# Ahead of the first MLP: the turns, the reciprocals and the value products one slot sooner, into the accumulators' banks

## What is computed

```python
scores = scale * np.matmul(q, k.transpose(0, 1, 3, 2))
kth = np.partition(scores, -top_k, axis=-1)[..., -top_k:-top_k + 1]   # top_k = 32
scores = np.where(scores >= kth, scores, -1000000000.0)
scores = scores - np.max(scores, axis=-1, keepdims=True)
attn = np.exp(scores)
attn = attn / (np.sum(attn, axis=-1, keepdims=True) + 1e-09)
x = np.matmul(attn, v)                                  # -> (2304, 512)
x = (sigmoid(x @ w_gate) * (x @ w_val)) @ w_out         # 512 -> 1536 -> 512
out = relu(x @ w_in) ** 2 @ w2_out                      # 512 -> 2048 -> 512
```

## Time and profile before

| | |
|---|---|
| median of 3 runs | 1231.99 us (1231.97 to 1233.85) |
| profiled execution | 1234.21 us, its span 1232.4 us |
| PE, busy in the span | 1164.7 us, 95% |
| DVE, busy in the span | 848.1 us, 69% |
| ACT, busy in the span | 740.2 us, 60% |
| POOL, busy in the span | 627.4 us, 51% |

### The profile page before, as it was taken

The page is one execution under the profiler, slowest core; times in us unless marked ns, Lnnn a source line. Parts: engine busy times, 40 slices in busy tenths (PEclk is TensorE's granted clock), DMA queues, the critical chain, the costliest instruction groups (busy, mean ns, idle before and its releaser), DMA issues.

```text
span 1232.4 us, 21820 instructions
## 1 busy us (share of the span) xinstructions
PE 1164.7 (95%) x7520; PEld 988.5 (80%) x7520; DVE 848.1 (69%) x1756; ACT 740.2 (60%) x1758; POOL 627.4 (51%) x539
## 2 busy tenths in 40 slices
PE   3459998999999999999999999999999999999999
PEld 1347887889988988888888777777777888888999
DVE  7988997978779967878997677788854544610121
ACT  5877777876778766656775665577554443621231
POOL 4865667766667745445663454356533342530220
PEclk9769999999999999999999999999999999999999
DMA  9874767677666685565556555545555455556997
GB/s 333 317 281 142 253 208 247 220 258 263 212 231 225 231 293 197 166 193 192 167 197 208 209 171 180 184 155 189 171 176 189 166 181 181 178 180 229 364 362 266
DMA packets 89245, 270.13 MB, mean 219 GB/s; under 512 B 9904, under 2 KB 15024, under 8 KB 89136
## 3 DMA queue, kind: packets, MB, share of 16 engines
q1 hardware_dynamic: 89136, 268.74, 63.8%
HBM read 228.33 MB, written 40.37 MB: 218 GB/s over the span
## 4 chain that ended last, share of the span: by engine, by line
PE 80%; ACT 8%; POOL 6%; DVE 3%; issue 2%; DMA 1%; SPq 0%; ACTq 0%; DVEq 0%; POOLq 0%
PE ps L553 21%; PE ps L555 20%; PE ps L554 20%; PE ps L494 7%; PE ps L458 5%; PE ps L474 5%; POOL below L784 3%; PE ps L539 3%; ACT scores L585 2%; DVE work L721 2%; DVE top L719 1%; ACT probs L604 1%; POOL stage L779 1%; ACT below L590 1%; ACT below L597 1%
## 5 line engine op out<-in xcount | busy, mean ns | idle before, releaser
L784 POOL TENSOR_TENSOR below<-scores,below 128x576 f32<-128x576 f32 x144 | 205.4, 1426 | 294.7 <-ACT below L597 291.6
L719 DVE MAX8 top<-work 128x8 f32<-128x576 f32 x432 | 313.0, 752 | 5.0
L553 PE MATMUL ps<-xy_hi,ring 128*128 128x512 f32 (+3 forms) x800 | 291.1, 364 | 0.0
L555 PE MATMUL ps<-xy_hi,ring 128*128 128x512 f32 (+3 forms) x800 | 282.8, 354 | 0.0
L554 PE MATMUL ps<-xy_lo,ring 128*128 128x512 f32 (+3 forms) x800 | 282.5, 353 | 0.0
L721 DVE MATCH_REPLACE8 work<-top,work 128x576 f32<-128x576 f32 x288 | 213.8, 743 | 0.0
L553 PE MATMUL ps<-g_hi,ring 128*128 128x512 f32 (+3 forms) x560 | 203.0, 362 | 0.0
L555 PE MATMUL ps<-g_hi,ring 128*128 128x512 f32 (+3 forms) x560 | 197.8, 353 | 0.0
L554 PE MATMUL ps<-g_lo,ring 128*128 128x512 f32 (+3 forms) x560 | 197.6, 353 | 0.0
L553 PEld LDWEIGHTS ps<-xy_hi,ring 128*128 128x128 f32 x800 | 150.8, 189 | 24.2 <-issue 9.4
L555 PEld LDWEIGHTS ps<-xy_hi,ring 128*128 128x128 f32 x800 | 150.8, 189 | 15.9
(11 more groups left out here) (58 smaller groups left out, 1734.5 us busy)
## 6 DMA issues: line engine op xcount, KB each, us to landing
ring<-w_split SPq DMA_DIRECT2D x318, 512.0 KB, 3.7
wring<-w_in SPq DMA_DIRECT2D x113, 256.0 KB, 4.0
w_split<-stage SPq DMA_DIRECT2D x46, 512.0 KB, 4.3
w_split<-ring SPq DMA_DIRECT2D x22, 512.0 KB, 2.9
vt<-v_in SPq DMA_DIRECT2D x16, 480.0 KB, 5.5
heads_in<-qk_in SPq DMA_DIRECT2D x16, 336.0 KB, 4.4
vt<-v_in SPq DMA_DIRECT2D x16, 320.0 KB, 3.9
heads_in<-qk_in SPq DMA_DIRECT2D x16, 240.0 KB, 4.0
```

Source lines behind the costliest of these rows:

```text
L553: nc.tensor.matmul(dst, w_hi, hi[:, k, 0:WIDTH[c]], start=first, stop=False)
L555: mm = nc.tensor.matmul(dst, w_lo, hi[:, k, 0:WIDTH[c]], start=False, stop=final)
L719: nc.vector.max(out=best, in_=sc if step == 0 else wk).then_inc(sel_step[t % 2], 1)
L784: nc.gpsimd.tensor_tensor(out=below[:, t % 2, :], in0=scores[:, t % PLACES, :], in1=below[:, t % 2, :], op=ALU.subtract).then_inc(mask_don ...
```

## The change

For tiles and units of chunk 0 only, the reciprocal and the normalising move from slot t+3 to t+2, the turn from END+3 to END+2, and the value product from END+4 to END+3. Their turned blocks go into banks 5, 6 and 7, which no MLP uses yet, so these turns no longer wait for copied scores or for the copied product of the unit before, and second-head scores no longer wait for them; the wait for the product moves to `times_v`. `MLP_AT` of chunk 0 becomes slot 15, while that of chunk 1 stays 41: 136 halves are spread over 26 slots where they were over 25.

Within a slot: in the prelude ScalarE now writes sign and enlarged sign ahead of the copy of scores, takes the exponential ahead of `copy_pt` (in slot 14 behind it), and the weight splits follow; 23 splits are spread over slots 0 to 13, one or two in each, and GpSimd does its part a slot later, between mask and normalise. VectorE's reciprocal stands behind the third pair of selection steps in the prelude, and from slot 15 on behind the second pair, where it stood behind the first. Later units keep their slots. The chunks are described by pieces of a batch; they hold the same tokens as before, but the outputs of chunks 3 and 4 are stored by two DMAs for each block of 128 features (8 DMAs more).

```diff
+PIECES = (((0, 0, 3),), ((0, 3, 6),), ((1, 0, 7),), ((1, 7, 2), (2, 0, 6)), ((2, 6, 3), (3, 0, 5)), ((3, 5, 4),))
...
-MASK, NORM, TURN, PROD = 2, 3, 3, 4
-MLP_AT = [CHUNK_END[c] + (5 if c < NW else 6) for c in range(NC)]
+MASK = 2
+MLP_AT = [CHUNK_END[c] + (4 if c == 0 else 6) for c in range(NC)]
+NORM_AT, TURN_AT, PROD_AT = {}, {}, {}
+for _t in range(NT):
+    _late = UNITS[TILES[_t][0]][0] > 0
+    NORM_AT[_t + 2 + _late] = _t
+    if _t in UNIT_AT:
+        TURN_AT[_t + 2 + _late] = PROD_AT[_t + 3 + _late] = UNIT_AT[_t]
...
-    SPLIT_AT.setdefault(min(2, MLP_AT[0] - (NPRE + 1) // 2) + _k // 2, []).append(_k)
+    SPLIT_AT.setdefault(_k * (MLP_AT[0] - 1) // NPRE, []).append(_k)
...
+        def turned(u, k, n):
+            bank = (5 if early(u) else 2) + k // 4
+            return ps[:, bank, P * (k % 4):P * (k % 4 + n)]
...
             def turn(u):
                 pe.wait_ge(norm_done, END[u] + 1)
                 wait(pe, pt_copied, u)
-                wait(pe, s_copied, max([t + 1 for t in range(NT) if TILES[t][1] == 1
-                                        and FIRST_OF[TILES[t][0]] - SCORE <= END[u] + TURN], default=0))
-                wait(pe, x_done, u)
+                if not early(u):
+                    wait(pe, s_copied, max([t + 1 for t in range(NT) if TILES[t][1] == 1
+                                            and FIRST_OF[TILES[t][0]] - SCORE <= TURN_SLOT[u]], default=0))
+                    wait(pe, x_done, u)
...
             def times_v(u):
                 pe.wait_ge(pt_copied, u + 1)
+                if early(u):
+                    wait(pe, x_done, u)
...
+            for s in range(min(SCORE_AT) + 1, MLP_AT[0]):
+                if 0 <= s - MASK:
+                    find_below(s - MASK)
+                    enlarge(s - MASK)
                 if s - 1 in SCORE_AT:
                     for t in tiles_of(SCORE_AT[s - 1]):
                         copy_scores(t)
+                if s in PROD_AT and s == MLP_AT[0] - 1:
+                    copy_pt(PROD_AT[s])
+                if 0 <= s - MASK:
+                    exp(s - MASK)
+                if s in PROD_AT and s < MLP_AT[0] - 1:
+                    copy_pt(PROD_AT[s])
+                for k in SPLIT_AT.get(s, []):
+                    split_weights(k)
+                if s in PROD_AT:
+                    copy_x(PROD_AT[s])
...
             for s in range(SLOTS):
-                select_both(s, [0])
-                if 0 <= s - NORM < NT:
-                    invert(s - NORM)
-                select_both(s, [1])
+                select_both(s, [0, 1])
+                if s in NORM_AT and s >= MLP_AT[0]:
+                    invert(NORM_AT[s])
                 for c, n in blocks_of(SHARES[s - 1][2]) if s else []:
                     evac(c, n)
                 select_both(s, [2])
+                if s in NORM_AT and s < MLP_AT[0]:
+                    invert(NORM_AT[s])
```

More of the change, by code:

```diff
@@ L23 @@
 KFULL = NBLK // 2
-CHUNK_BLOCKS = (3, 6, 7, 8, 8, 4)
-NC = len(CHUNK_BLOCKS)
+PIECES = (((0, 0, 3),), ((0, 3, 6),), ((1, 0, 7),), ((1, 7, 2), (2, 0, 6)), ((2, 6, 3), (3, 0, 5)), ((3, 5, 4),))
+NC = len(PIECES)
 NW = 1
-WIDTH = [B64 * n for n in CHUNK_BLOCKS]
-START = [sum(WIDTH[:c]) for c in range(NC)]
+WIDTH = [sum(B64 * n for b, at, n in pieces) for pieces in PIECES]
 NMAX = max(WIDTH)
@@ L36 @@
 for _c in range(NC):
-    _at, _end = START[_c] // B64, (START[_c] + WIDTH[_c]) // B64
-    while _at < _end:
-        _n = min(_end, (_at // NBLK + 1) * NBLK) - _at
-        GROUPS += [(_c, _at // NBLK, _p, _at % NBLK, _n, B64 * _at - START[_c]) for _p in range(PAIRS)]
-        _at += _n
+    _col = 0
+    for _b, _at, _n in PIECES[_c]:
+        GROUPS += [(_c, _b, _p, _at, _n, _col) for _p in range(PAIRS)]
+        _col += B64 * _n
 NG = len(GROUPS)
@@ L351, in wait_stored, with stores_ahead @@
                 eng.wait_ge(ring_stored[ring_place(k)], 16 * ring_stores(k))
+        def stores_ahead(c, m):
+            ahead = sum(len(PIECES[i]) for i in range(min(c, NC))) * (NM // 2)
+            return 16 * (ahead + (len(PIECES[c]) * (m // 2) if c < NC else 0))
         block = ctx.enter_context(nc.Block())
@@ L425, in _ @@
                     load_v(V_AT[s])
+                for k in SPLIT_AT.get(s - 2, []):
+                    load_weights(k + WPLACES)
                 for k in SPLIT_AT.get(s - 1, []):
-                    load_weights(k + WPLACES)
-                for k in SPLIT_AT.get(s, []):
                     store_parts(k)
@@ L443, in score @@
                 wait(pe, s_copied, FIRST_OF[u])
-                if part == 1:
-                    wait(pe, pt_copied, sum(END[v] + TURN < FIRST_OF[u] - SCORE for v in range(NU)))
+                ahead = sum(TURN_SLOT[v] < FIRST_OF[u] - SCORE for v in range(NU))
+                if part == 1 and ahead and not early(ahead - 1):
+                    pe.wait_ge(pt_copied, ahead)
                 q = B64 * GROUPS[g][4]
@@ L569, in _ @@
                         score(t)
-                if s - PROD in UNIT_AT:
-                    times_v(UNIT_AT[s - PROD])
+                if s in PROD_AT:
+                    times_v(PROD_AT[s])
                 for c, h in SHARES[s][1] + SHARES[s][2]:
                     mlp_half(c, h)
-                if s - TURN in UNIT_AT:
-                    turn(UNIT_AT[s - TURN])
+                if s in TURN_AT:
+                    turn(TURN_AT[s])
             for c, h in REST:
@@ L653, in evac @@
                         else:
-                            wait(act, out_stored[t], 16 * c * NM // 2)
+                            wait(act, out_stored[t], stores_ahead(c, t))
                         nc.scalar.activation(act_buf[:, t % 2, 0:n_w], acc(c, n), ACT.Tanh,
@@ L664, in evac @@
                     elif kind == "out":
-                        wait(act, out_stored[t % 2], 16 * (c * NM // 2 + t // 2))
+                        wait(act, out_stored[t % 2], stores_ahead(c, t))
                         nc.scalar.activation(act_buf[:, t % 2, 0:n_w], acc(c, n), ACT.Copy).then_inc(out_copied, 1)
@@ L678, in _ @@
             nc.scalar.activation(rsum_eps[:, 0:1], ident[:, 0:1], ACT.Exp)
-            for s in range(min(SCORE_AT) + 1, SLOTS):
+            for s in range(min(SCORE_AT) + 1, MLP_AT[0]):
+                if 0 <= s - MASK:
+                    find_below(s - MASK)
+                    enlarge(s - MASK)
                 if s - 1 in SCORE_AT:
@@ L834, in _ @@
                     mask(s - MASK)
-                if 0 <= s - NORM < NT:
-                    normalise(s - NORM)
+                for k in SPLIT_AT.get(s - 1, []):
+                    split_weights(k)
+                if s in NORM_AT:
+                    normalise(NORM_AT[s])
                 for c, n in blocks_of(SHARES[s - 1][2]) if s else []:
@@ L840, in _ @@
                     split_x(c, p)
-                for k in SPLIT_AT.get(s, []):
-                    split_weights(k)
                 for c, n in blocks_of(SHARES[s][0] + SHARES[s][1]):
```

56 lines of the change are left out of this document (32 added, 24 removed).

## The result

| | before | with the change |
|---|---|---|
| median | 1232.93 us (1231.97 to 1233.85, 6 runs) | 1241.47 us (1239.92 to 1242.96, 6 runs) |
| profiled execution, its span | 1234.21, 1232.4 us | 1239.92, 1238.1 us |

The ratio is 1.007, with a 95% interval of 1.0057 to 1.0083: the change makes the kernel slower by 8.5 us. The forecast was 1229.2 and its range ended at 1233.0. The profiled execution with the change is its fastest one, and that of before is slower than all six of its runs, so the traces show only 5.7 of the 8.5 us.

What follows compares the result with a forecast made beforehand. TensorE sets the pace, VectorE nearly full, and ScalarE paces the prelude. First MLP 3.8 us earlier, 1.0 lost, 2.8 won by chunk 1's MLP, the other edits nothing; span 1232.4 to 1229.6, median forecast 1229.2 us, range 1225.0 to 1233.0.

Steps and rivals of the forecast that it cites:

- The splits cost nothing: Prelude: weight splits keep their count and go to the stores a slot earlier; nothing, unless a load comes late.
- A round of 18.6 to 19.4 us: Prelude: ScalarE's time for three slots with the change, 18.6 taken, where it was 17.58.
- the catch: Prelude: only splits, at most 1.14 us, now cover a product of 2.08 to 2.40, so ScalarE waits for TensorE.
- The first MLP's start as the measure: First matmul of chunk 0's MLP: about 92.1 us against 95.91, taken as 3.8 us earlier.
- The wait of 5.93 us: Late prelude: unit 6's turn stands 5.93 us for scores to leave its banks; the change was to lose this.
- Five halves fewer are 3.4 us, of which 1.0 is lost: First MLP from slot 17: 12 halves done and not 7; of TensorE's 3.8 us lead, 2.8 survives until slot 41.
- rival C: First MLP: its slots are paced by VectorE and ScalarE, so nothing is won; 1232.0 us, chance 0.20.
- Beyond chunk 1's MLP the same length: From chunk 1's first MLP matmul to the end: 987 us as now, wrong if moved by over 1 us.
- The reciprocal: VectorE's reciprocal one pair of passes later, 2 x 0.74 us: with the row sum's gain nothing, 0.5 us either way.
- rival B: Prelude: the whole slot is won, TensorE keeps the fast clock, rotating banks lets copies overlap; 1226.4 us, chance 0.20.
- Rival D: First MLP: thinner work makes TensorE stand longer and its clock fall, 3.6 us per event; 1235.6 us, chance 0.10.
- Rival E: Prelude: unit 7's product is sooner by number, not time; rounds of 19.4, MLP at 94.5; 1231.3 us, chance 0.08.

Runs made afterwards that it cites:

- e1: The changed kernel with no weight split in slot 2, the fifth and later ones spread over slots 3 to 13; 1238.22 us, ratio 1.0039.
- e5: e3 with ScalarE copying turned blocks ahead of the exponential in all prelude slots; 1233.67 us, ratio to before 1.0007.
- e3: The changed kernel with the edits of both e1 and e2; 1238.17 us, ratio to before 1.0041.
- e6: e3 with the first MLP from slot 16 on again, 136 halves over 25 slots; 1237.62 us, ratio to before 1.0040.
- e8: e3 with ScalarE's copies of scores behind sign and enlarge also in slots 15 to 38; 1227.67 us, ratio to before 0.9957.
- e2: The changed kernel with loads of queries, keys and values ahead of the leftover MLP DMAs in slot 40; 1239.87 us, ratio to before 1.0059.
- e7: The kernel before with chunk 0's turned blocks in banks 5 to 7 and the needless waits removed; 1230.32 us, ratio 0.9982.
- e10: e7 with copies of scores behind sign and enlarge in slots 16 to 38; 1226.00 us, ratio to before 0.9952.
- e12: e10 with that order of the copies of scores from slot 2 on; 1222.57 us, ratio to before 0.9925.
- e11: The kernel before with only the copies of scores behind sign and enlarge in slots 16 to 38; 1228.64 us, ratio 0.9973.
- e4: The changed kernel with VectorE's reciprocal behind the first pair of selection steps again from slot 15 on; 1240.44 us, ratio to before 1.0065.
- e9: e5 with e8's edit, copies of scores behind enlarge in slots 15 to 38; 1226.05 us, ratio to before 0.9954.

## Why the prediction was wrong

**The splits cost nothing: failed, by 3.2 us.** The prediction gave this edit nothing "unless a load comes late". It looked at loads; what was late was a store, which holds the place that the fifth split writes. Slot 4 is at 27.50 and not at 24.3. e1 takes that away: slot 4 at 23.76, and 3.2 us of the median.

**A round of 18.6 to 19.4 us, with the catch: held.** From slot 4 to 7, 10 and 13 the rounds take 18.7, 19.3 and 19.0, together 1.2 more than 3 x 18.6; slot 13 takes 6.8 and not 8.0, 1.2 less; from the sign of slot 14 to the MLP it is 4.0, as forecast. 92.1 + 3.2 + 1.2 - 1.2 = 95.3, the measured start. e5 shows the catch at 4.5 us.

**The first MLP's start as the measure: failed.** The prediction said that the change can act on that start and on how the time behind it is filled. It compared 92.1 with 95.91 and called it 3.8 us ahead. But the change's MLP starts a slot number earlier, while chunk 1's MLP stays in slot 41, so what counts is when slot 16 comes. The prediction's own 88.1 for the sign of slot 14 held that answer: the trace of before has it at 84.41, 3.7 us sooner. e3, which meets the forecast times, is in slot 16 at 98.08 against 97.21. The wait of 5.93 us that the prediction took off was not won with the change either: the turn of unit 6 stands 5.74 us for its own input.

**Five halves fewer are 3.4 us, of which 1.0 is lost: failed, and with it the whole gain of 2.8 us.** This was rival C's mechanism; C named VectorE and ScalarE and argued it from VectorE's busy time. TensorE's work was not the bound: from slot 17 at 103.26 e3 takes 142.8 us to chunk 1's MLP, where the forecast had 242.7 - 102.9 = 139.8 and the kernel before, with five halves more, took 142.2. TensorE stands 11.1 us there, where it stood 7.8: the five halves turned into standing. e6 puts them back and loses nothing; e8 changes only ScalarE's order and wins 7.0 us from slot 16 to slot 41, some 1.4 of them by the clock. The prediction looked at VectorE's lead over TensorE and took busy shares for pace; ScalarE, at 76 to 77% in the first window, was the pacer, by its wait for GpSimd inside each slot. The same 1.52 us stood in the earlier trace rows, and the prediction used it for the prelude and not for the slots behind.

**Beyond chunk 1's MLP the same length: failed.** 990.1 against 986.9, and 2.6 of that is standing. The order of the loads explains 2.2 of it in the traces of e2 and e3, and at most 1.6 in the medians; the other 1 us is open. The rests of the other kernels differ by the clock too: e2, e3, e5, e7, e10 and e12 have a stretch at the lower clock between 380 and 405 us and TensorE is busy 979.6 to 980.1 us in the rest; in the others it is 978.0 to 978.7. Among the traces without such a stretch, before and e11 have a rest of 986.9 and 986.2, and e4, e6, e8 and e9, which are built on the change and have its eight extra output DMAs, 987.4 to 988.4. So some 1 us seems to belong to the change behind chunk 1's MLP, and no run shows to which part of it: none took the DMAs out alone.

**The reciprocal: held** within what e4 can tell. **The banks** as such were right, and rival B's rule with them, but they are worth 2.4 us and only without the rest of the change.

**Rival D** was right that the change is slower, and not by its mechanism: the stretch at the lower clock that it looked for between 100 and 245 did not come, and the one of before is gone (1.00 and 1.00 in the windows above, 1.00 and 0.97 in the earlier trace rows). One event at the start of the MLP is told below; it isn't what decides. **Rival E** had the right shape, slots that are sooner by number and not by time, but took the MLP's start as its measure as well. Its sign, a start above 94, came by the store and not by its rounds of 19.4.

**What turned the sign.** In the trace chunk 1's MLP starts 5.3 us later than forecast and the rest is 3.2 us longer. The gain of 2.8 did not come, and by rival C's sum that alone gives no change. Slower it became by the store, 3.2 us (e1), by a prelude whose slots come later (the catch, 4.5 us by e5, was in the forecast's rounds but not in its measure), and by the longer rest.

The account from before to the change, in medians: banks -2.4 (e7), the slot earlier with the new order and 26 slots +3.3 (e7 to e5), the copy behind the exponential +4.5 (e5 to e3), the store and the loads +3.3 (e3 to the change; e1 gives 3.2 to the store). That is +8.7 against 8.5 measured; as each step is the difference of two medians, the sum had to come out, and it confirms nothing. The second term holds several edits, and no run divided it.

## What to carry to other kernels

When work is moved "a slot sooner", compare the time at which the same slot number comes, not the start of the moved work: the later stations stay at their numbers. Where an engine executes in order and waits for another in every iteration, put independent work into that wait, and look for such a pacer by its waits, not by its busy share. Before work is brought forward, ask of each buffer that it writes when its last store went out and behind which transfers. And when a pacer is taken away, look again at what was worth nothing: here the halves of TensorE's work.

## What the runs showed of the hardware

The clock answers the same gap in two ways. With the change TensorE stands 2.75 us ahead of the last product of the prelude, and the first eight rows of the MLP take 2.62 us; in e1 it stands 2.80 and the same eight take 1.57. The windows of that stretch, the change and then e1:

```profile
95.70:99.10 3.40, 3.40 (x14) 2.69 (x14) 3.21 (x8) 1.89 (x4) 2.00 (x2) 0.50 0.82 278
```

```profile
92.30:95.70 3.40, 3.40 (x37) 2.62 (x37) 3.40 (x9) 2.42 (x7) 1.80 (x2) 1.00 0.47 157
```

The granted clock is at its lower level, 1.2 GHz, in one and at 2.4 GHz in the other. It cost 1.05 us on the MLP's rows and 0.58 on the scores behind them (1.82 against 1.24). The same is seen at a turn near 400 us, in e3 and then with the change:

```profile
396.20 1.58 PE L502 MATMUL ps<-ident,probs 128*128 128x128 f32 x9 [1.94 <-ACT scores L616]
```

```profile
401.05 1.17 PE L500 MATMUL ps<-ident,probs 128*128 128x128 f32 x9 [2.04 <-ACT scores L614]
```

Behind 1.94 us of standing the turn and the eight matmuls after it run at the lower clock (0.52 us for most of them, where they take 0.33; the granted clock is 0.75 from 394.0 to 400.8). Behind 2.04 us they do not (1.00 from 399.0 to 405.8). Such an event in one trace is no trait of a kernel: executions of one kernel here spread over 3 us, and e8's first MLP starts 1.8 us later than e3's, though nothing ahead of it differs.

A store of 512 KB among the first loads has another price than one later: the four issued between 12.79 and 19 us took 8.9 us to landing in the median, against 4.6 over all 46.
